# Attention, routed experts and a dense layer in one kernel: expert tiles reordered, weight parts spread over them, weights sent further ahead

## The reference

```
scores = where(is_sink | in_window, q @ k.T / 8, -1e9)
x   = softmax(scores) @ v                       # rows (3072, 512)
take = x @ w_skip > 0                           # the others pass unchanged
e    = argmax(x @ w_gate);  gate = softmax(x @ w_gate)[e]
x[take] += gate * (relu(x @ w1[e]) @ w2[e])     # w1 512x1024, w2 1024x512
out = relu(x @ w_in)**2 @ w_out                 # w_in 512x2048, w_out 2048x512
```

## Time and profile before

| | before |
|---|---|
| median of 3 runs | 1062.45 us |
| the profiled execution | 1068.57 us |
| its span | 1066.9 us |
| PE busy | 995.2 us (93%) |
| DVE busy | 443.3 us (42%) |
| ACT busy | 413.4 us (39%) |
| attention | 0 to 240 us |
| experts | 254 to 499 us |
| dense layer | 511 to 1066 us |

### The profile page before, as it was taken

The page is one execution under the profiler, slowest core; times in us unless marked ns, Lnnn a source line. Parts: engine busy times, 40 slices in busy tenths (PEclk is TensorE's granted clock), DMA queues, the critical chain, the costliest instruction groups (busy, mean ns, idle before and its releaser), DMA issues.

```text
span 1066.9 us, 16107 instructions
## 1 busy us (share of the span) xinstructions
PE 995.2 (93%) x5432; PEld 803.1 (75%) x5433; DVE 443.3 (42%) x1337; ACT 413.4 (39%) x953; POOL 62.5 (6%) x105
## 2 busy tenths in 40 slices
PE   7999999973998989897999999999999999999998
PEld 5777777762776868675788888888888888888886
DVE  5666666755554535355432322322232132223223
ACT  6777666661454544343432222222132122113122
POOL 2011111111110111110000000000000000000000
PEclk9999999976998989998899999999999999999999
DMA  4444555217154555551500200020020002002001
GB/s 164 141 140 125 167 196 189 67 51 284 55 210 195 215 212 212 204 195 60 209 1 1 80 1 1 1 79 0 0 79 0 0 0 79 0 0 79 0 0 39
DMA packets 33711, 99.45 MB, mean 93 GB/s; under 512 B 5261, under 2 KB 5261, under 8 KB 31360
## 3 DMA queue, kind: packets, MB, share of 16 engines
q1 hardware_dynamic: 27792, 86.27, 23.0%
q0 software_dynamic: 4720, 10.69, 2.9%
q10 hardware_dynamic: 1152, 1.90, 0.5%
HBM read 77.97 MB, written 25.82 MB: 97 GB/s over the span
## 4 chain that ended last, share of the span: by engine, by line
PE 73%; DVE 9%; DMA 6%; issue 6%; ACT 4%; DVEq 1%; POOL 0%; POOLq 0%; SPq 0%; ACTq 0%
PE bank L904 25%; PE bank L918 25%; PE bank L847 5%; DMA x_res<-routed 4%; PE bank L831 4%; PE bank L756 3%; DVE w_lo L301 3%; PE bank L729 2%; PE bank L778 2%; DVE score L977 2%; ACT prob L554 2%; PE bank L703 1%; PE bank L767 1%; DVE xT_a L1083 1%; PE bank L886 1%
## 5 line engine op out<-in xcount | busy, mean ns | idle before, releaser
L1175 DVE TENSOR_TENSOR g<-relu_c 128x512 f32<-128x512 f32 x96 | 66.4, 692 | 362.8 <-ACT relu_c L649 362.7
L649 ACT ACTIVATE relu_c<-bank 128x512 f32<-128x512 f32 x96 | 57.4, 598 | 386.5 <-PE bank L904 386.5
L904 PE MATMUL bank<-x_hi,w_lo 128*128 128x512 f32 x384 | 152.7, 398 | 0.9 <-DVE x_lo L1168 0.9
L918 PE MATMUL bank<-w_hi,g_lo 128*128 128x512 f32 x384 | 153.0, 399 | 0.0
L904 PE MATMUL bank<-x_hi,w_hi 128*128 128x512 f32 x384 | 153.0, 399 | 0.0
L904 PE MATMUL bank<-x_lo,w_hi 128*128 128x512 f32 x384 | 152.8, 398 | 0.0
L918 PE MATMUL bank<-w_hi,g_hi 128*128 128x512 f32 x384 | 152.0, 396 | 0.0
L918 PE MATMUL bank<-w_lo,g_hi 128*128 128x512 f32 x384 | 151.8, 395 | 0.0
L554 ACT ACTIVATE prob<-score,neg_max 128x264 f32<-128x264 f32 (+1 forms) x192 | 93.5, 489 | 28.1 <-DVE neg_max L977 26.8
L301 DVE TENSOR_TENSOR w_lo<-w_raw,w_hi 128x1024 fp32r<-128x1024 f32 x80 | 92.3, 1219 | 3.7 <-ACT w_hi L296 3.6
L904 PEld LDWEIGHTS bank<-x_hi,w_lo 128*128 128x128 f32 x384 | 72.7, 189 | 19.0 <-issue 1.2
(11 more groups left out here) (119 smaller groups left out, 1364.1 us busy)
## 6 DMA issues: line engine op xcount, KB each, us to landing
w_raw<-in_weights SPq DMA_DIRECT2D x18, 2048.0 KB, 13.8
x_c<-x_rows SPq DMA_DIRECT2D x28, 256.0 KB, 3.6
k_in<-in_kT SPq DMA_DIRECT2D x24, 264.0 KB, 3.9
q_in<-in_qT SPq DMA_DIRECT2D x24, 256.0 KB, 3.1
v_in<-in_v SPq DMA_DIRECT2D x24, 256.0 KB
x_rows<-x_row SPq DMA_DIRECT2D x24, 256.0 KB, 2.6
out<-w_raw SPq DMA_DIRECT2D x12, 512.0 KB, 2.8
x_raw<-routed SPq DMA_DIRECT2D x18, 260.0 KB
```

The source lines that it names most:

```text
L649: eng.activation(relu_c[:, f % 2, :], hc_ps[f % 2][:, :], ACT.Relu).then_inc(s_crelu, 1)
L904: ins = eng.matmul(hc_ps[f % 2][:, :], w[f // UNIT][:, f % UNIT, wcols], x[:, c, :], start=(c == 0 and n == 0), stop=(c == DC - 1 and n == 2))
L918: ins = eng.matmul(yc_ps[s][:, :], gg[:, f % 2, s * P:(s + 1) * P], w[f // UNIT][:, f % UNIT, DM:CH], start=(f == 0 and n == 0), stop=(f = ...
L1175: eng.tensor_tensor(g[:, f % 2, :], relu_c[:, f % 2, :], relu_c[:, f % 2, :], ALU.mult).then_inc(s_cg, 1)
```

## The change

It does five things. (1) Unit 0's w_hi is made by ACT in steps 13 to 20 of attention, one chunk in each, ahead of expl; its w_lo by DVE in steps 14 to 21, behind the reciprocals; SP loads the raw chunks two steps earlier. (2) SP loads unit e+2 in expert e (and unit 1 in step 24 of attention), the front half when chunk 3 of unit e+1's w_lo is made, the back half when chunk 7 is; the load stands where the old one stood in SP's program, so the x_raw loads behind it wait too. (3) In the first tile of an expert ACT makes chunks 0 to 3 at once, waits for PE's end of the tile before (s_by), makes 4 and 5, then one behind relu_b(0) and one behind x_upper; DVE makes 0 to 2 ahead of hb_lo(0), 3 behind it, 4 behind xb_lo, and 5 to 7 behind hb_lo(1). (4) Layer 2 takes the hb_lo terms last, and turn_h(1) stands behind two blocks of three matmuls instead of one. (5) The row counts for the padding are copied to the table in the last `count`, with a semaphore of their own, s_padrow, and DVE waits for the constants in step 2.

```diff
@@ upper_chunk: each chunk of unit 0 has its own semaphore @@
-                nc.scalar.wait_ge(s_w0, 16 * UNIT)
+                nc.scalar.wait_ge(s_w0[f], 16)
@@ SP @@
             def load_w(u):
                 for half, cols in ((0, slice(0, UNIT // 2)), (1, slice(UNIT // 2, UNIT))):
+                    eng.wait_ge(s_wlo, u * UNIT - UNIT // 2 * (1 - half))
+                    if not isinstance(u, int):
+                        close(eng)
                     eng.dma_start(w_raw[:, cols, :], weights[bass.ds(u, 1), :, cols, :].rearrange("o p c d -> (o p) c d")).then_inc(s_w[half], 16)
...
-                if i >= TILES - UNIT - 4 and i < TILES - 4:
-                    f = i - (TILES - UNIT - 4)
-                    eng.dma_start(w_raw[:, f, :], weights[0, :, f, :]).then_inc(s_w0, 16)
+                if i == TILES:
+                    load_w(1)
+                if i >= TILES - UNIT - 6 and i < TILES - 6:
+                    f = i - (TILES - UNIT - 6)
+                    eng.dma_start(w_raw[:, f, :], weights[0, :, f, :]).then_inc(s_w0[f], 16)
...
-            eng.wait_ge(s_table, 1)
+            eng.wait_ge(s_padrow, 1)
             store_padding(eng, (0,), s_pad0)
...
             eng.wait_ge(s_pad0, 16)
+            eng.wait_ge(s_table, 1)
             eng.sem_inc(s_bgo, 1)
...
             def expert(e, slot, first, end):
                 load_rows(first + 1, second_tile(eng, e))
-                parts_made(eng, e)
-                load_w(e + 1)
+                load_w(e + 2)
                 with eng.If(first + 2 < end):
                     with eng.Fori(first + 2, end) as n:
                         load_rows(n, later_tile(eng, e, first, n))
...
-            parts_made(eng, E)
-            load_w(E + 1)
@@ ACT @@
-                if i >= TILES:
-                    for f in range(3 * (i - TILES), min(3 * (i - TILES) + 3, UNIT)):
-                        upper_chunk(0, 0, f)
+                if i >= TILES - UNIT - 3 and i < TILES - 3:
+                    upper_chunk(0, 0, i - (TILES - UNIT - 3))
...
+            eng.wait_ge(s_padrow, 1)
+            store_padding(eng, range(1, E), s_pad)
             eng.wait_ge(s_table, 1)
-            store_padding(eng, range(1, E), s_pad)
...
+                chunks(range(0, DC))
+                if make is not None:
+                    eng.wait_ge(s_by, n + 1)
+                chunks(range(4, 6))
                 relu_b(0)
-                chunks(range(0, 1))
+                chunks(range(6, 7))
                 h_upper(0)
                 relu_b(1)
                 x_upper(n + 1)
-                chunks(range(1, 2))
+                chunks(range(7, 8))
                 h_upper(1)
-                chunks(range(2, UNIT))
             def expert(e, slot, first, end):
-                eng.wait_ge(s_by, first + 1)
                 tile(e, first, 1 - slot)
@@ PE @@
-                def layer2(chunks):
+                def layer2(chunks, terms):
                     for c in chunks:
                         at = slice(c % 4 * P, c % 4 * P + P)
                         cols = slice(c % 2 * DM, c % 2 * DM + DM)
-                        for k, (h, w) in enumerate(((hb_hi, w_lo[slot]), (hb_lo, w_hi[slot]), (hb_hi, w_hi[slot]))):
+                        for k in terms:
+                            h, w = ((hb_hi, w_lo[slot]), (hb_hi, w_hi[slot]), (hb_lo, w_hi[slot]))[k]
+                            if k == 2 and c % 4 == 0:
+                                eng.wait_ge(s_bhlo, n * 2 + c // 4 + 1)
                             ins = eng.matmul(y_ps[:, :], h[:, c // 4, at], w[:, DC + c // 2, cols],
                                              start=(c == 0 and k == 0), stop=(c == FC - 1 and k == 2))
...
                 eng.wait_ge(s_brow, n + 1)
-                eng.wait_ge(s_bhlo, n * 2 + 1)
-                layer2((0,))
+                eng.wait_ge(s_bhhi, n * 2 + 1)
+                layer2((0, 1), (0, 1, 2))
                 turn_h(1)
-                layer2((1, 2, 3))
-                eng.wait_ge(s_bhlo, n * 2 + 2)
-                layer2((4, 5, 6, 7))
+                layer2((2, 3), (0, 1, 2))
+                eng.wait_ge(s_bhhi, n * 2 + 2)
+                layer2((4, 5, 6, 7), (0, 1))
+                layer2((4, 5, 6, 7), (2,))
@@ DVE @@
                 def count():
                     eng.tensor_tensor(carry[:, :], route_ps[:, COUNT:COUNT + E], carry[:, :], ALU.add).then_inc(s_route, 1)
+                    if j == TILES - 1:
+                        eng.wait_ge(s_route, TILES)
+                        eng.tensor_copy(table[:, 2 * E:3 * E], carry[0:1, :]).then_inc(s_padrow, 1)
...
-            eng.wait_ge(s_const, 7)
             for i in range(TILES + 3):
                 a, bb, c, d = step_flags(i)
+                if i == 2:
+                    eng.wait_ge(s_const, 7)
...
                 if bb:
                     reciprocals(i - 1)
+                if i >= TILES - UNIT - 2 and i < TILES - 2:
+                    lower_chunk(eng, 0, 0, i - (TILES - UNIT - 2))
...
             eng.wait_ge(s_table, 1)
-            for f in range(UNIT):
-                lower_chunk(eng, 0, 0, f)
...
+                chunks(range(0, 3))
                 h_lower(0)
+                chunks(range(3, 4))
                 x_lower(n + 1)
+                chunks(range(4, 5))
                 h_lower(1)
-                if make is not None:
-                    for f in range(UNIT):
-                        lower_chunk(eng, e + 1, make, f)
+                chunks(range(5, 8))
```

More of the change, by code:

```diff
@@ L199, in build @@
         s_scatter = [sem(f"s_scatter{n}") for n in range(3)]
-        s_tchain, s_table = sem("s_tchain"), sem("s_table")
-        s_w0 = sem("s_w0")
+        s_tchain, s_table, s_padrow = sem("s_tchain"), sem("s_table"), sem("s_padrow")
+        s_w0 = [sem(f"s_w0{n}") for n in range(UNIT)]
         s_w = [sem(f"s_w{n}") for n in ("_front", "_back")]
@@ L845, in layer2 @@
                         cols = slice(c % 2 * DM, c % 2 * DM + DM)
-                        for k, (h, w) in enumerate(((hb_hi, w_lo[slot]), (hb_lo, w_hi[slot]), (hb_hi, w_hi[slot]))):
+                        for k in terms:
+                            h, w = ((hb_hi, w_lo[slot]), (hb_hi, w_hi[slot]), (hb_lo, w_hi[slot]))[k]
+                            if k == 2 and c % 4 == 0:
+                                eng.wait_ge(s_bhlo, n * 2 + c // 4 + 1)
                             ins = eng.matmul(y_ps[:, :], h[:, c // 4, at], w[:, DC + c // 2, cols],
                                              start=(c == 0 and k == 0), stop=(c == FC - 1 and k == 2))
-                    if chunks[-1] == FC - 1:
+                    if chunks[-1] == FC - 1 and terms[-1] == 2:
                         ins.then_inc(s_by, 1)
@@ L1124, in _ @@
             eng.tensor_copy(table[:, E:2 * E], cnt[:, 3, :])
-            eng.scalar_tensor_tensor(out=table[:, 3 * E:4 * E], in0=region0[0:1, :], scalar=float(P), in1=carry[0:1, :], op0=ALU.add, op1=ALU.min)
-            eng.tensor_copy(table[:, 2 * E:3 * E], carry[0:1, :]).then_inc(s_table, 1)
+            eng.scalar_tensor_tensor(out=table[:, 3 * E:4 * E], in0=region0[0:1, :], scalar=float(P), in1=carry[0:1, :], op0=ALU.add, op1=ALU.min).then_inc(s_table, 1)
             eng.wait_ge(s_table, 1)
-            for f in range(UNIT):
-                lower_chunk(eng, 0, 0, f)
             def x_lower(n):
@@ L1141, in h_lower, with chunks @@
                     eng.tensor_tensor(hb_lo[:, half, :], hT_ps[half][:, :], hb_hi[:, half, :].bitcast(F32), ALU.subtract).then_inc(s_bhlo, 1)
+                def chunks(which):
+                    for f in which if make is not None else ():
+                        lower_chunk(eng, e + 1, make, f)
+                chunks(range(0, 3))
                 h_lower(0)
+                chunks(range(3, 4))
                 x_lower(n + 1)
+                chunks(range(4, 5))
                 h_lower(1)
-                if make is not None:
-                    for f in range(UNIT):
-                        lower_chunk(eng, e + 1, make, f)
+                chunks(range(5, 8))
                 eng.wait_ge(s_by, n + 2)
```

## The result

The changed kernel takes **1097.5 us** (median of 4 runs, 1097.4 to 1103.77) against 1061.86 us for the kernel before beside it (4 runs, 1060.17 to 1064.88). The ratio is **1.0347, with a 95% interval of 1.0303 to 1.0391**: slower, by about 36 us. The forecast was 1064 us with 1036 to 1076 as its range. The profiled execution took 1097.42 us (span 1095.7), which is its median; that of before had been nearly 7 us above its own, so between the two profiles only 28.8 us of span are to be found.

A forecast was written before the change was run, and what follows sets the result against it. It took PE's waits in the expert stage (31.5 us lost, mostly for hb_lo) and attention's loop through all engines as the bounds; terms summed to +1.9 us on the 1062.45 us median, giving 1064 us, range 1036 to 1076.

The forecast's parts named there:

- What is late next: Expert stage: x_raw queues behind the weights' back half, PE waits 2.5 us at turn_x per expert; +27.2 with the clock.
- The clock: Expert stage: slow matmuls after each x_raw gap, 0.9 us per gap on the mean, +7.2 over eight.
- The old stalls: Expert stage: PE's waits, mostly for hb_lo, all go with weights one unit ahead and parts spread: -30 us.
- Attention: Eight w_hi chunks ahead of expl +7.6; constants waited for later -0.9; w_hi gone from the tail -0.5.
- The padding row: Before the experts: earlier padding store lets x_raw go sooner, -0.9; bounds 0 (last scatter becomes late) and -2.5.
- The start of the dense layer: Last stage: x_c's last two loads no longer share with weights, so PE's second x_c wait goes: -0.6.
- The expert tiles: No late engine in a first tile; 17 tiles take 212.7 us, plus 1.5 us for the half-clock beginning.
- Rival 1: Expert stage: x_raw is in time because small loads overtake or chunk 7 is early; -25.3, 1037 us, chance 0.17.
- Rival 2: Expert stage: the x_raw gaps are there but the clock holds; -7.2, 1057 us, chance 0.15.
- the rule that stood beside it: Skill's rule: only long idle gaps bring the clock down, so 2.5 us gaps are free; sum would be -5.3.
- Rival 3: Attention: the clock falls inside the loop, 3.2 us per such step; +13 at four steps, 1077 us, chance 0.15.
- Rival 4: Expert stage: weight load stays beside x_res and PE still waits at layer 2; near 1066 us, chance 0.03.

The follow-up runs named there:

- experiment 7: Kernel after with 18 unread filling matmuls ahead of turn_x in every tile but an expert's first: 1090.11 us, ratio 1.0257.
- experiment 9: Kernel before with only the attention part of the change (unit 0's parts made inside attention, w_hi ahead of expl): 1072.88 us, ratio 1.0111.
- experiment 10: Kernel before with only the attention part, its w_hi chunk moved into ACT's wait ahead of turned(i, 0): 1060.95 us, ratio 0.9999.
- experiment 3: Kernel after with ACT's w_hi chunk in attention moved from ahead of expl into ACT's wait ahead of turned(i, 0): 1089.33 us, ratio 1.0261.
- experiment 4: Kernel after with x_raw issued ahead of the weights and the w_hi chunk in ACT's gap: 1035.67 us, ratio 0.9745.
- experiment 1: Kernel after with SP's weight load moved behind the x_raw load of the next expert's first tile: 1044.35 us, ratio 0.9832.
- experiment 2: Kernel after with x_raw issued between the weights' two halves, still after the wait for chunk 7: 1046.19 us, ratio 0.9854.
- experiment 11: Kernel after with nine unread filling matmuls ahead of turn_x in every tile but an expert's first: 1093.51 us, ratio 1.029.
- experiment 6: Kernel after with the back half of the weights cut into two loads of 1 MB: 1093.53 us, ratio 1.0288.
- experiment 5: Experiment 4 with the old expert tiles: w_hi and w_lo chunks in one block, old layer 2 order: 1051.54 us, ratio 0.9899.
- experiment 8: Experiment 4 with layer 2's terms and turn_h(1) in the order of the kernel before: 1039.2 us, ratio 0.9778.

## Why the prediction was wrong

**The step that failed is "What is late next", by the size of its gap and of the clock's price.** The +27.2 us of that step measured 36.8 + 15.8 = 52.6. The mechanism was the one forecast, term by term: chunk 7 ends 13.25 us into the expert's first tile (384.98 - 371.73, the start of that tile's layer 1), SP issues the back half 0.95 us into the second, x_raw queues behind it, and PE stands at turn_x once in each of eight experts. But the gap was 4.6 us for 2.5, outside even its bounds of 0 to 4: **16.8 us more**. Of the 2.1 us per gap, 0.9 came before the issue (x_raw left 1.9 us into the tile, 0.97 behind the back half, where I had counted nothing for it) and 1.2 on the way (8.71 us for the 7.5 of the sum). The 1.2 are the size of a slip in my own sum: an x_raw load alone takes 3.55 us, and without the 0.7 for its bytes 2.85 are left for starting and landing, not the 1.6 that I wrote. With 2.85 the way is 8.75 us. That this meets the 8.71 is luck in part, for I had sent 2.1 MB at 401 GB/s through empty engines, and they moved 263 to 387 GB/s and had the end of the front half and a scatter to carry too. The nearest rows were in my hands and were passed over: four x_c loads that landed after 9.3 to 9.9 us behind a 4 MB weight load issued 5.6 us before them; here the front half went out 6.9 us before x_raw (at 379.30). They give issue at 1.0 plus 9.3 to 9.9, a landing 10.3 to 10.9 us into the tile and a gap of 4.3 to 4.9, above my upper bound; measured are 10.6 and 4.6.

**The clock** cost 15.8 us for 7.2, 2.0 per gap for 0.9: **8.6 us more**. The mean over two gaps, one of them free, mixed two outcomes: behind a gap the clock falls and costs 1.3 to 2.7 us, or it holds and the gap costs nothing more. At 4.6 us it fell behind all eight, at 2.5 us behind five of eight (1.3 us on the mean), in experiment 7 behind none of seven. The row with the slow stretch alone (1.6 us) would have given 8 x 1.6 = 13 us.

**The old stalls** were put at -30, read from the one profiled execution. In it they were nearly that: 244.1 - 215.0 = 29.1. But that execution was 6.7 us above the median, and experiments 9 and 10 ran the same tiles in 241.0 and 238.0 us. So 23 to 26 us is what those executions had to give, and by carrying the difference to the median I counted 4 to 7 us that were not there. With the two sums above and 1 us of attention this makes 30 to 34 of the 33.5 us between 1064 and 1097.5.

**Attention** was right in its large term: 7.3 us longer for 7.6 - 0.9 - 0.5 = 6.2, steps of 10.66 us with a chunk. The eight chunks cost 7.7 us, but the constants gave back 0.1 for 0.9 (the first expl comes at 33.99 us for 34.10: the wait of the earlier trace rows is gone and ACT waits for DVE elsewhere) and the tail 0.3 for 0.5. What the prediction missed was that the price was one of place and not of work (experiments 3, 4 and 10).

**The padding row** came out in number and by luck: the stretch from the last rank matmul to the experts is 0.8 us shorter for 0.9. In the chain of waits of the kernel after x_raw now waits for the last scatter, which was the case of its bound 0:

```profile
250.14 4.44 DMA routed<-x_row,slot_i
```

So x_raw is issued only 0.15 us earlier behind the rank matmul (7.37 us for 7.52). The rest is its landing, 3.24 us for 3.55, and 0.3 us from there to the first tile. **The start of the dense layer** came out: PE's second wait for x_c is 0.30 us for 0.63, and the stretch ahead of the first product 12.3 us for 12.8 (forecast -0.6).

**The expert tiles** were right: no engine is late in them (experiments 1 and 2), and the undisturbed stage is 215.0 us for 212.7 + 1.5.

**The rivals.** Rival 1 is what experiment 1 builds, and it is real: without the queueing the kernel gains (1044.35 us for its 1037). The 7 us between fit the 4 to 7 counted too much for the old stalls and the 1.4 by which attention was longer there than in the kernel after. It did not happen by itself, since no load overtook the weights. Rival 2 (gaps, but the clock holds) is refuted at the length it spoke of: experiment 11 has gaps of 2.5 us and half speed behind five of eight. By that, the rule that stood beside it (the Trainium skill, TensorE: Matmul & The Clock Gate, "HAM oscillation — how this bites in real kernels") did not hold for gaps of this length here. Rival 3, the clock falling inside attention, was not the cause, but it is alive. The window from 20 to 225 us, PE alone (stretch, busy, granted clock, DMA share, GB/s), first in experiment 6, then in the kernel after:

```profile
20.00:225.00 205.00, 190.85 (x1719) 0.96 0.42 136
```

```profile
20.00:225.00 205.00, 189.56 (x1775) 1.00 0.43 137
```

With w_hi ahead of expl attention ran at 0.96 to 0.99 in the profiled executions of experiments 1, 2, 6, 7 and 9 and at 1.00 in 11 and after. It cost 1.4 to 3.7 us where attention took 249.0 to 251.3 us for 247.6, not the 13 of the rival. With the chunk in ACT's gap (3, 4, 5, 8, 10) it was 1.00 each time. That the added idle time in PE's loop causes it is what this pattern suggests; no run isolated it. Rival 4 is refuted by the waits of after.

## What to carry to other kernels

When a load gets a new wait, or goes further ahead, price every small load behind it in the same queue's program by the slowest landing that the trace shows behind such a load, not by bytes over bandwidth; and put the small load first: that one line was worth 53 us here. A copy of a microsecond that is free in one idle place costs its full length in another of the same step, so look for the engine's wait inside the loop before placing it. Behind a gap count the full price of the half clock or nothing, each with a chance, and not their mean. And read the size of a stall from more than one execution where the clock takes part in it.

## What the runs showed of the hardware

**A small load waits for the large one ahead of it.** x_raw (260 KB) took 8.1 to 9.0 us to land behind 2 MB on SP's queue in the kernel after, and 3.24 us alone between the stages. Issued ahead of the 2 MB, 1.3 us into the tile for 1.9 (experiment 2), it was in time. The Trainium skill (DMA: Bandwidth & Descriptors, "Queues, rings and completion order") has descriptors consumed in ring order, and a semaphore's increment landing only behind the earlier writes of the same DMA engine, from any queue. The late landings here fit it; no run looked into a single DMA engine's queue. Another queue does not help by itself: x_res (260 KB), on GpSimd's queue beside SP's weights, took up to 11.9 us to land in experiment 5 and 2.9 at best. No run sent x_raw itself through another queue.

**Cutting the load finer helps little** (experiment 6: gaps of 3.9 for 4.6 us with the last piece halved). In the kernel after the engines were busy 0.84 to 0.99 of the time from the front half on, so there was little to win.

**A gap costs the half clock or nothing, and its length changes how often.** Where the matmul stream on both sides is the same, 1.2 GHz followed all eight gaps of 4.2 to 4.9 us (the kernel after) and all eight of 3.0 to 4.8 (experiment 6), five of the eight of 2.0 to 3.2 us (experiment 11) and none of the seven of 0.2 to 2.0 us (experiment 7). When the clock fell it cost 1.3 to 2.7 us, whatever the length. Between 2.0 and 3.3 us both happen: 2.02 us was free in experiment 7 and 3.31 us in the kernel before, 1.97 us in experiment 11 and 2.02 us in the kernel before were not the earlier trace rows. What decides between two such gaps stays open.
